# Moving the chunk places that carry no attention unit, and the gate's rank products, in a fused attention, MLP and expert kernel

## The reference

```python
# 1. attention, batch 4, heads 8, seq 768, head_dim 64; 4 sink columns, window of 128
scores = scale * np.matmul(q, k.transpose(0, 1, 3, 2))
scores = np.where(is_sink | in_window, scores, -1e9)
a = softmax(scores)                      # with 1e-9 on the sum
x = (a @ v) laid out as 3072 tokens x 512
# 2. MLP, 512 -> 2048 -> 512
h = x @ w_in
g = h - np.tanh(h)
x = g @ w_out
# 3. eight experts, one for each token, 512 -> 1024 -> 512
logits = x @ w_gate + modality_bias[modality_id]
e_idx = np.argmax(logits, axis=1); gate_w = softmax(logits)[e_idx]
out[mask] = gate_w[mask, None] * (np.maximum(x[mask] @ w1[e], 0.0) @ w2[e])
```

## Time and profile before

| what | value |
|---|---|
| time, median of 3 runs | 1098.25 us (1096.22 to 1101.44) |
| the profiled execution's own time | 1100.37 us |
| its span from first to last instruction | 1098.8 us |
| TensorE busy in the span | 92% |
| VectorE, ScalarE, GpSimd busy | 65%, 56%, 36% |
| TensorE's mean granted clock | 0.975 of full |

### The profile page before, as it was taken

How to read it: one execution, slowest core, us unless ns; L and a number is a source line. 1 busy time by engine, 2 the same in 40 slices (tenths; PEclk the granted TensorE clock), 3 DMA queues, 4 the chain that set the end, 5 groups by cost and what they waited for, 6 DMA issues and landing times.

```text
span 1098.8 us, 24366 instructions
## 1 busy us (share of the span) xinstructions
PE 1005.4 (92%) x7840; PEld 631.2 (57%) x7840; DVE 712.1 (65%) x2464; ACT 613.2 (56%) x1425; POOL 400.1 (36%) x462
## 2 busy tenths in 40 slices
PE   1668988998999999899999899999999999999996
PEld 0434544565555565555555556555476777677774
DVE  6677957677977877887787786655765334643331
ACT  2777867575777666668576576645522224532221
POOL 3788775322335322424333232011024222232322
PEclk9967999999999999999999999999999999999998
DMA  9843111241312331231132130014023311111111
GB/s 278 284 111 69 36 35 35 72 118 35 64 35 55 51 121 35 38 95 35 35 64 60 44 64 2 1 52 160 1 30 121 138 43 47 52 39 48 48 48 37
DMA packets 24844, 75.15 MB, mean 68 GB/s; under 512 B 9712, under 2 KB 10096, under 8 KB 23216
## 3 DMA queue, kind: packets, MB, share of 16 engines
q1 hardware_dynamic: 15856, 60.58, 20.8%
q0 software_dynamic: 5728, 13.43, 3.8%
q10 hardware_dynamic: 3168, 0.02, 0.1%
HBM read 60.16 MB, written 14.12 MB: 68 GB/s over the span
## 4 chain that ended last, share of the span: by engine, by line
PE 64%; DVE 14%; issue 6%; ACT 6%; POOL 5%; DMA 2%; DVEq 1%; SPq 0%; ACTq 0%; POOLq 0%
PE h_ps L728 15%; PE acc L784 15%; PE pt_ps L1811 10%; PE h_ps L1862 5%; PE acc L1862 5%; PE x_out L683 3%; PE pt_ps L629 2%; PE s_ps L560 2%; DVE qk_top L399 2%; PE x_out L687 2%; DVE g_raw L749 2%; PE s_ps L835 1%; DVE g_lo L769 1%; DMA qk_raw<-in_qk 1%; POOL kl_stack L450 1%
## 5 line engine op out<-in xcount | busy, mean ns | idle before, releaser
L784 PE MATMUL acc<-w_out_all,g_hi 128*128 128x512 f16 x768 | 231.1, 383 | 0.0
L728 PE MATMUL h_ps<-xt_hi,w_in_all 128*128 128x384 f16 x960 | 196.9, 328 | 11.4 <-DVE g_raw L749 10.9
L784 PE MATMUL acc<-w_out_all,g_lo 128*128 128x512 f16 x384 | 147.2, 383 | 8.4 <-DVE g_lo L769 6.9
L612 ACT ACTIVATE pt_hi<-pt_ps 128x256 f16<-128x256 f32 (+2 forms) x224 | 83.1, 378 | 101.3 <-PE pt_ps L629 99.0
L728 PEld LDWEIGHTS h_ps<-xt_hi,w_in_all 128*128 128x128 f16 x960 | 91.3, 98 | 81.8 <-DVE g_raw L749 15.1
L769 DVE SCALAR_TENSOR_TENSOR g_lo<-g_raw,batch_scale,g_hi 128x384 f16<-128x384 f32 x128 | 96.5, 754 | 35.8 <-ACT g_hi L759 34.3
L784 PEld LDWEIGHTS acc<-w_out_all,g_hi 128*128 128x128 f16 x768 | 75.6, 98 | 71.2 <-issue 2.5
L99 POOL TENSOR_TENSOR tick<-tick 1x1 f32<-1x1 f32 x83 | 15.7, 190 | 274.1 <-ACT y L1878 115.6
L616 DVE TENSOR_TENSOR pt_lo<-pt_ps,pt_hi 128x256 f16<-128x256 f32 (+2 forms) x224 | 94.4, 423 | 30.3 <-ACT pt_hi L612 28.2
L450 POOL TENSOR_TENSOR q_stack<-qk_raw,q_stack 64x768 f16<-64x768 f32 x31 | 50.8, 1638 | 162.1 <-ACT q_stack L446 162.1
L740 ACT ACTIVATE g_raw<-h_ps,batch_scale 128x384 f32<-128x384 f32 x120 | 69.5, 579 | 63.0 <-PE h_ps L728 58.0
(11 more groups left out here) (312 smaller groups left out, 2125.6 us busy)
## 6 DMA issues: line engine op xcount, KB each, us to landing
qk_raw<-in_qk SPq DMA_DIRECT2D x62, 454.0 KB, 6.0
raw<-in_w SPq DMA_DIRECT2D x16, 512.0 KB, 9.0
v_raw<-in_v SPq DMA_DIRECT2D x4, 1536.0 KB, 9.9
x_tokens<-x SPq DMA_DIRECT2D x24, 256.0 KB, 6.1
w_in_all<-in_w_in SPq DMA_DIRECT2D x4, 1024.0 KB, 14.7
w_out_all<-in_w_out SPq DMA_DIRECT2D x4, 1024.0 KB, 12.0
x_tokens<-g_raw SPq DMA_DIRECT2D x1, 1024.0 KB, 14.0
qk_raw<-in_qk SPq DMA_DIRECT2D x2, 262.0 KB, 4.4
```

What stands on the lines that cost most here:

```text
L612: eng.activation(pt_hi[:, at, :], out, ACT.Copy).then_inc(q["pt_hi_done"], 1)
L728: mm = eng.matmul(h_of(m, f), w16[0][:, f, x * DM + k * P:x * DM + (k + 1) * P], r[:, par, k, :], start=(i == 0), stop=(i == 3 * KD - 1))
L784: mm = eng.matmul(acc[t][:, :], l[f % 2][:, t * P:(t + 1) * P], w16[1][:, f, x * DM:(x + 1) * DM], start=(f == 0 and i == 0), stop=(f == N ...
```

## The change

Two numbers are edited. In windows 1 to 7 the rests move from places 1, 4, 6, 7, 19, 20, 22, 26 to 4, 5, 10, 11, 16, 17, 25, 26. For the gates of chunks 0 to 5 all four parts of `gate_rank` come one place later (26 to 29 in place of 25 to 28); the gate of chunk 6 (`g == NC - 2`), in window 7, stays at 27. Window 0 and the number of units of each window are as before.

```diff
@@ gate_slot
             if 20 <= k < 25:
                 gate_choose(E, eng, g, (k - 20,))
-            at = 27 if g == NC - 2 else 25
+            at = 27 if g == NC - 2 else 26
             if at <= k < at + 4:
                 gate_rank(E, eng, g, (k - at,))
@@ window
-                rest = k in ((13, 17, 19, 22, 30, 31) if w == 0 else (1, 4, 6, 7, 19, 20, 22, 26))
+                rest = k in ((13, 17, 19, 22, 30, 31) if w == 0 else (4, 5, 10, 11, 16, 17, 25, 26))
                 n = 10 ** 6 if rest else i
```

## The result

| | before | after |
|---|---|---|
| median of 6 runs each | 1101.0 us (1096.22 to 1102.05) | 1091.24 us (1087.26 to 1093.83) |
| profiled execution | 1100.37 us, span 1098.8 | 1091.96 us, span 1090.4 |

The ratio is 0.9933, interval 0.991 to 0.9957: some 7.4 us faster (4.7 to 9.9), where 13.0 were forecast. The time lies inside the range, the direction is right, the size is not.

A forecast was written before the change was run, and what follows sets the result against it. TensorE, busy 92% of the span, was taken as the bound, so only its waits count: 6.3 + 2 x 1.2 + 3.1 - 0.4 + 1.6 = 13.0 us, from 1098.25 to 1085 us; range 1082 to 1097.

The forecast's parts named there:

- The rank wait: Windows 1 to 5: the rank products' wait (L887) for the scores' reading goes, 10.4 us, before VectorE's work falls due elsewhere.
- Windows 1, 3, 5: Places 21 to 26: a wait of 1.1 us before `mlp_in` of 24 replaces 3.2; gain 2.1 us each, 6.3 in all.
- The knife edge: Windows 1, 3, 5: L864 starts some 0.1 us sooner, ahead of GpSimd's L450, and is taken as free instead of held.
- The copies and `normed`: Windows 2 and 4: rests at 11, 16 and 17 remove the waits for the gate's copy and `normed`; gain 3.1 us.
- Places 0 to 5: Windows 2 and 4: `mlp_in` of place 6 waits about 0.9 us where place 2 waited 0.46; loss 0.4 together.
- Windows 2 and 4, the same places: Places 21 to 26: L864 stays free, L867 becomes free; waits of 1.0 to 1.3 replace 2.5; gain 1.2 us each.
- The clock: Window 4, place 25: the clock drop after the rank wait no longer occurs; 1.6 us come back.
- case A: The main forecast, L864 free in windows 1, 3, 5: 13.0 us gained, 1085 us, chance 0.50.
- Rival D: Slower by clock: waits of 1.8 and 1.4 us in windows 1 to 5 each bring a 1.57 us drop; 1109, chance 0.10.
- case B: L864 held by GpSimd in windows 1, 3, 5, which then gain nothing: 6.7 us gained, 1091.5 us, chance 0.25.
- C: No change: units at 18 to 24 and 0 to 3 undo the rests' gain through VectorE's backlog; 1094 to 1100, chance 0.15.

The follow-up runs named there:

- e1: The kernel before with only the rank products moved one place later (25 to 26), rests as before: 1090.41 us, ratio 0.9946 to the kernel before.
- e2: The kernel before with only the new rests, rank products left at place 25: 1091.55 us, ratio 0.9944 to the kernel before.
- e4: The change plus a one-element VectorE store, awaited, ahead of L864 in windows 1 to 5: 1095.86 us, ratio 1.0001 to the kernel before.
- e3: The change with only L864 (addition of `iota_e`) issued one place earlier: 1086.42 us, ratio 0.9897 to the kernel before; 1083.58 us in its repeat.
- e9: e3 with L865 and L867 moved to the rest 25 and choose part 4 to the rest 26: 1080.28 us, ratio 0.9839 to the kernel before.
- e8: e3 with the first two rests put back from 4, 5 to 1, 4: 1090.18 us, ratio 0.9929 to the kernel before.
- e5: e1 with L864 one place earlier, so without the new rests: 1088.69 us, ratio 0.9902 to the kernel before.
- e7: e3 with the rest of place 16 moved to 22: 1093.07 us, ratio 0.9955 to the kernel before.

## Why the prediction was wrong, step by step

**Right.** *The rank wait* went (9.5 shown to none), and e1 and e2 show that either edit alone removes it. *Windows 1, 3, 5*: 2.06, 2.07 and 2.21 us won, 2.1 each forecast; the one wait left at places 21 to 26 is 1.02 shown before `mlp_in` of 24 in window 1, 1.2 by starts, 1.1 forecast. *The knife edge* there: L864 went ahead of GpSimd by 0.09, and e4 shows that the margin was real and what its other side costs. *The copies and `normed`*: 2.1 shown fell to 0.3, two of 0.17 where none was forecast. *Places 0 to 5*: window 2's `mlp_in` of place 6 waits 0.85 by starts, 0.9 forecast.

**The step that failed** is "*Windows 2 and 4, the same places.* L864 was free there and L867 held". I carried over from before that L864 is free, and asked only where L867 would land. But place 20 has become a unit's place there too. VectorE stood idle for 1.09 us between L862 and `mlp_gate` of place 21 before, and now not at all; L862 itself took 0.18 before and 0.59 now, held by GpSimd's L488 (344.16). What follows came later against GpSimd's, and L864 went from 0.12 ahead of L450 to 0.04 behind. The hold of L862 alone may be enough for that. It cost 0.41 us and VectorE had no pause from there to L864; some 0.2 of it would reach L864, since `g_lo` began at 346.94 and ScalarE's `g_hi` was ready at 346.71. That is an estimate from these rows: no run moved L862, and it took 0.59 in e3 and 0.58 in e9 too. The margin of window 1 I worked out; the margin of window 2, of the same size, I did not. It gave waits of 0.9 and 2.0 us in place of the 1.0 to 1.3 in all. e3 takes away the hold of L864, and with it that of L867 (0.74 and 0.59), and brings the two windows from 92.55 and 90.73 to 89.09 and 88.78: 5.4 us, nearly all of the 5.7 between the forecast of 13.0 and the 7.3 in the windows (windows 1, 3, 5 give 0.2 each more). Even so `mlp_in` of 24 waits 0.8 and 1.0 by starts in e3, where 0.5 was forecast, and the further 0.5 forecast behind place 25 doesn't come. The sum of e3 is 13.4 below that of before.

**The clock** failed with it. "No single wait of case A is above 1.3" did not hold in window 2 or 4, and in window 2 the drop came, some 1.5 us of the 5.4. The 1.6 of window 4 did come back. The size of the longest wait was no safe sign either: in e8 the clock fell behind a wait of 1.05. Rival D had the mechanism, and e4 shows it in windows 1, 3 and 5, where the waits of case B are followed by a clock of 0.64 and 0.62.

**The rivals.** B was the right mechanism in the wrong windows. The Trainium skill (SBUF — State Buffer, "SBUF: two separate sides") has it that whoever starts first keeps the shared pair for the whole instruction. The rows agree in all windows: 0.18 when 0.09 ahead, 1.69 when 0.04 behind, 2.19 when 0.01 behind. C, that the new rests bring nothing beside the rank shift, is true of the change as it stands (e1 has 525.6 against its 526.0), though its time, 1094 to 1100, was not met. C's reason, that VectorE's backlog cancels the rests, is neither shown nor ruled out. With L864 early the kernel with the new rests is 4.4 us faster (e3 against e5), but e5 still has a hold, that of L867, and how much of the 4.4 is the rests' own is not shown. What they do take away by themselves are the waits for the copies and `normed` (2.1 shown to 0.3).

**Still open**: when the clock falls. Shown waits of 0.73 to 1.08 and then 1.82 to 1.83 stand in windows 2 and 4 of the change, of e2 and of e4, six times in all, and only window 2 of the change has the drop. Nothing here tells it from the other five, so of the 5.7 us missing some 1.5 may be there in one execution and not in the next. Why e9's last 0.4 to 0.5 before `mlp_in` of 24 stays was not tried.

## What to carry to other kernels

Where the profile shows a small VectorE instruction as long as a GpSimd one beside it, write down which of the two starts first in every kind of window, with the margin, and price an edit for both orders wherever the margin is 0.1 to 0.2 us; better, move the small instruction out of reach first, since that alone was worth 6 us here. Then look at which instruction comes next to GpSimd's in its place: with the rests of before the hold only passed on to L867. Two edits that remove the same wait don't add up, and what one of them costs elsewhere then shows as a change that brings only half. Steps of 0.2 us whose result is not wanted at once belong where VectorE has a rest, not ahead of the instruction for which TensorE waits.

## What was not expected of the hardware

- The hold depends on 10 to 90 ns: 24 elements took 0.18 us when begun 0.09 ahead of GpSimd's split, 2.19 when begun 0.01 after it. In window 4 of e3, L867 began 0.02 ahead of GpSimd's L521 and took 0.17.
- It isn't only for two inputs in SBUF: L862, one tensor by a constant, took 0.59 (in the change) and 1.60 us (in e7) behind GpSimd and ended within 0.04 of it both times. The reduction L865 (0.18 at 350.19, while GpSimd's L513 ran from 350.10) and the scale steps on one element (0.15 each inside L450 in window 1) were not held.
- A hold is in no list of waits: it lengthens the held instruction, and TensorE's wait is put down to whatever came last behind it (`neg_max`, `g_raw`).
- The same two waits in a row, some 2.55 us shown together, were followed by a clock of 0.67 in window 2 and of 1.00 in window 4 of one execution; one wait of 1.05 in e8 by 0.62 in window 2 and 1.00 in window 4. In e4's windows 1, 3 and 5, 1.71 and 1.26 were followed by 0.64, 0.62 and 0.62.
